# Attention in 80 tile steps placed inside the chunks of two gated convolutions, on one core

## The chip, the core and the metric

One core of a Trainium2 chip runs the whole program. The time is device microseconds from the first to the last instruction. The engines are TensorE (PE, with its weight loads as PEld), VectorE (DVE), ScalarE (ACT), GpSimd (POOL) and SyncE (SP), which only issues transfers. Each runs its own instruction list in order and waits on semaphores.

## What is computed

Windowed attention with a linear bias, then two gated convolution blocks. All data is float32.

```python
# q, k, v: 4 batches, 8 heads, 576 rows, 64 columns; a row sees itself and the 127 rows before it
scores = scale * q @ k.T - slope[h] * distance, masked
attn = exp(scores - max) / (sum + 1e-9);  x = (attn @ v) as (4, 576, 512)
# block 1: 3 taps over h, centred
h = relu(x @ w_in)                        # 512 -> 1024
x = (h * sigmoid(conv3(h))) @ w_out       # 1024 -> 512
# block 2: 5 taps over x, looking back 4 rows
y = ((x @ w_val) * sigmoid(conv5(x))) @ w_out2
```

## The kernel before

The program has two stages, one after the other.

**Attention.** A step is 128 query rows of one pair of heads: 4 batches x 4 pairs x 5 tiles = 80 steps. The fifth tile of a pair (t = 4) has 64 rows only, and the first (t = 0) has fewer keys. A full step is: PE `scores` (L756, two products of 192 columns), DVE `scores` (L582: takes the product out of PSUM, adds the bias and finds the maximum), ACT `exps` (L408, exponential with its sum), DVE `guard` (L596), `invert` (L605) and `normalise` (L614), PE `turn` (L777, four transposes), ACT or DVE `copy_out` (L422, L626), PE `mix` (L808, L805: the product with v). Scores run 5 steps ahead. After a pair's five tiles ACT copies the result from PSUM to `x_all` (L433, L430). The bodies are loops over three batches and one written out.

During this stage POOL takes the twelve 512 KB weight panels, each as it lands: it rounds one into `w_hi` (L345) and subtracts to get `w_lo` (L348), through two buffers `w_raw`.

**The convolutions.** The 2304 rows of x are cut into 8 chunks of 288 rows. For each, PE runs four products, and each block of 128 x 128 weights is used three times (hi x hi, hi x lo, lo x hi, L839 to L841; L893 to L895 in chunk 0): `up` (8 blocks m of 12 products), `val` of the chunk before (4 x 12), `down` (4 x 24), `out` of the chunk before (4 x 12): 288 products. Between `up` and `down` each of the eight blocks m passes ACT `hidden_rows` (L464), DVE three taps (L668, L672), ACT sigmoid (L470), DVE `gated` (L680), ACT rounding to `g1_hi` (L479), POOL subtraction to `g1_lo` (L370). `hidden` and `conv` have DEPTH = 4 buffers, and tap 0 of block m + 1 is issued between taps 1 and 2 of block m. After `down` DVE runs the second block's five taps (L702, L706), and `val_rows` (L690) multiplies by the gate. Before each chunk ACT rounds its 290 columns of `x_all` to `x_hi` (L450) and POOL subtracts (L356). `up` and `down` use PSUM banks 0 to 3, `val` and `out` banks 4 to 7. The first sigmoid needs a load of ACT's function table; the exponential has one at the program's start.

## Time and profile before

| | us |
|---|---|
| median of 3 runs (485.01 to 489.94) | 488.39 |
| span of the profiled execution | 489.8 |
| PE / PEld busy | 453.4 / 415.2 |
| DVE / ACT / POOL busy | 370.8 / 247.8 / 177.9 |

The profile lists instructions with start and duration. A DVE or ACT duration contains some fixed time that overlaps the next instruction, so that the distance between two starts is the better measure of cost. "Idle before" is what the engine stood still, with the name of what ended it. PEclk is the clock that TensorE was granted: 1.00 is its upper level of 2.4 GHz, 0.50 its lower level of 1.2 GHz.

### The profile page before, as it was taken

To read this page: it belongs to the slowest core of one execution; us is meant where nothing else is said; L and a number is where in the kernel's file an instruction comes from. 1 tells how busy PE (TensorE), PEld (TensorE's weight loads), DVE (VectorE), ACT (ScalarE), POOL (GpSimd) and SP (SyncE) were. 2 spreads that over 40 slices of the span, in tenths; PEclk is the share of its full clock that TensorE was granted. 3 is DMA by queue.
4 is the path that set the end of the run, shared out by engine and by line. 5 is a ranking of instruction groups with operands and counts; after the bars stand their busy time and mean duration, and the time that the engine had idled before them with its cause. 6 is when DMAs were issued, how large, how long until landed. Compare 5 with 4: busy or idle time off the path is not lost.

```text
span 489.8 us, 10856 instructions
## 1 busy us (share of the span) xinstructions
PE 453.4 (93%) x3424; PEld 415.2 (85%) x3424; DVE 370.8 (76%) x1078; ACT 247.8 (51%) x746; POOL 177.9 (36%) x181
## 2 busy tenths in 40 slices
PE   4989788887889998999999999999999999999997
PEld 3767566665667897998999999999999999999996
DVE  5889967787767586896696786977968769669750
ACT  3777656775748563354354355255344344435432
POOL 2223522243310026157148136326425605713611
PEclk9999979998879998999999999999999999999999
DMA  5465435433413000000100000010010010010011
GB/s 146 116 176 149 148 106 168 154 115 115 141 49 98 1 2 0 2 1 1 50 1 1 32 17 0 12 36 0 0 48 0 0 48 0 0 48 2 1 48 50
DMA packets 37626, 25.52 MB, mean 52 GB/s; under 512 B 20704, under 2 KB 34016, under 8 KB 37600
## 3 DMA queue, kind: packets, MB, share of 16 engines
q1 hardware_dynamic: 37600, 25.20, 17.1%
q8 instruction: 14, 0.23, 0.2%
q14 instruction: 12, 0.10, 0.1%
HBM read 20.47 MB, written 4.72 MB: 51 GB/s over the span
## 4 chain that ended last, share of the span: by engine, by line
issue 33%; PE 28%; DVE 17%; POOL 16%; ACT 2%; DMA 1%; POOLq 1%; DVEq 0%; SPq 0%; ACTq 0%; PEldq 0%
POOL g_lo L370 10%; PE bank L756 7%; PE bank L777 7%; PE bank L808 5%; DVE guarded L596 4%; POOL x_lo L379 4%; DVE probs L614 3%; DVE conv L672 3%; PE bank L839 2%; PE bank L841 2%; PE bank L840 2%; POOL g_lo L362 2%; DVE gate L706 2%; DVE conv L680 1%; DVE probs L582 1%
## 5 line engine op out<-in xcount | busy, mean ns | idle before, releaser
L839 PE MATMUL bank<-x_hi,w_hi 128*128 128x290 f32 (+1 forms) x384 | 113.8, 296 | 0.5 <-ACT hidden L464 0.5
L840 PE MATMUL bank<-x_lo,w_hi 128*128 128x290 f32 (+1 forms) x384 | 113.7, 296 | 0.0
L841 PE MATMUL bank<-x_hi,w_lo 128*128 128x290 f32 (+1 forms) x384 | 113.7, 296 | 0.0
L839 PE MATMUL bank<-g_hi,w_hi 128*128 128x288 f32 x352 | 105.4, 300 | 3.2 <-POOL g_lo L370 1.7
L370 POOL TENSOR_TENSOR g_lo<-conv,g_hi 128x288 fp32r<-128x288 f32 x64 | 60.2, 949 | 131.2 <-ACT g_hi L479 131.2
L840 PE MATMUL bank<-g_lo,w_hi 128*128 128x288 f32 x352 | 103.9, 295 | 0.0
L841 PE MATMUL bank<-g_hi,w_lo 128*128 128x288 f32 x352 | 103.6, 294 | 0.0
L706 DVE SCALAR_TENSOR_TENSOR gate<-x_all,taps,gate 128x288 f32<-128x288 f32 x128 | 80.7, 630 | 4.5
L672 DVE SCALAR_TENSOR_TENSOR conv<-hidden,taps,conv 128x288 f32<-128x288 f32 x128 | 83.4, 657 | 0.6
L839 PEld LDWEIGHTS bank<-x_hi,w_hi 128*128 128x128 f32 x384 | 72.3, 188 | 0.8 <-ACT hidden L464 0.8
L840 PEld LDWEIGHTS bank<-x_lo,w_hi 128*128 128x128 f32 x384 | 72.8, 189 | 0.0
L841 PEld LDWEIGHTS bank<-x_hi,w_lo 128*128 128x128 f32 x384 | 72.5, 189 | 0.0
L408 ACT ACTIVATE probs<-probs,neg_max 128x192 f32<-128x192 f32 (+1 forms) x144 | 62.1, 434 | 20.2 <-DVE neg_max L582 19.2
L839 PEld LDWEIGHTS bank<-g_hi,w_hi 128*128 128x128 f32 x352 | 66.1, 188 | 6.8 <-POOL g_lo L370 5.7
L582 DVE CUSTOM_DVE_ANT_0 probs<-bank,bias 128x192 f32<-128x192 f32 (+1 forms) x144 | 46.5, 324 | 31.3 <-PE bank L756 22.0
L756 PE MATMUL bank<-k_pair,q_heads 128*128 128x192 f32 (+2 forms) x288 | 63.3, 345 | 6.9 <-DMA k_pair<-k_t 6.9
L777 PE MATMUL bank<-identity,probs 128*128 128x128 f32 x256 | 48.8, 306 | 20.4 <-DVE probs L614 20.2
L841 PEld LDWEIGHTS bank<-g_hi,w_lo 128*128 128x128 f32 x352 | 66.2, 188 | 0.0
L840 PEld LDWEIGHTS bank<-g_lo,w_hi 128*128 128x128 f32 x352 | 66.1, 188 | 0.0
L777 PEld LDWEIGHTS bank<-identity,probs 128*128 128x128 f32 x256 | 28.5, 149 | 35.2 <-DVE probs L614 24.1
L470 ACT ACTIVATE conv<-conv 128x288 f32<-128x288 f32 x64 | 28.5, 445 | 54.8 <-DVE conv L672 54.8
L756 PEld LDWEIGHTS bank<-k_pair,q_heads 128*128 128x128 f32 x288 | 49.4, 214 | 7.0 <-issue 6.8
(55 smaller groups left out, 670.8 us busy)
## 6 DMA issues: line engine op xcount, KB each, us to landing
w_raw<-panels SPq DMA_DIRECT2D x12, 512.0 KB, 4.2
q_heads<-q_t SPq DMA_DIRECT2D x32, 144.0 KB, 3.1
k_pair<-k_t SPq DMA_DIRECT2D x16, 288.0 KB, 3.7
y_t<-y_sb SPq DMA_DIRECT2D x32, 144.0 KB, 1.8
v_pair<-v_pairs SPq DMA_DIRECT2D x16, 256.0 KB, 2.7
v_pair<-v_pairs SPq DMA_DIRECT2D x16, 32.0 KB, 2.5
taps<-taps SPq DMA_DIRECT2D x1, 12.0 KB, 3.6
taps<-taps SPq DMA_DIRECT2D x1, 10.0 KB, 3.9
```

Of the source, the lines that this page charges most:

```text
L370: pool.tensor_tensor(g1_lo[:, m, :], conv[m % DEPTH][:, :], g1_hi[:, m, :], ALU.subtract).then_inc(g1_lo_done, 1)
L408: last = act.activation(probs[r][:, half, lo:hi], probs[r][:, half, lo:hi], ACT.Exp, bias=neg_max[r][:, half:half + 1], scale=-1.0, accum_ ...
L470: act.activation(conv[m % DEPTH][:, :], conv[m % DEPTH][:, :], ACT.Sigmoid).then_inc(gate1_done, 1)
L582: last = dve.tensor_tensor_reduce(probs[r][:, half, lo:hi], s[:, 2 * P * half + lo:2 * P * half + hi], bias_of(hp, t, half), -SCALE, 3e38, ...
L672: dve.scalar_tensor_tensor(out=out, in0=rows, scalar=taps1[:, tap, m:m + 1], in1=out, op0=ALU.mult, op1=ALU.add).then_inc(tap1_done if tap ...
L706: dve.scalar_tensor_tensor(out=out, in0=x2_all[:, m, at + tap:at + tap + HALF], scalar=taps2[:, tap, m:m + 1], in1=out, op0=ALU.mult, op1= ...
L756: last = pe.matmul(s[:, 2 * P * half + lo:2 * P * half + hi], q[:, 2 * t + half, :, :], k[:, first_key + lo:first_key + hi], start=True, s ...
L777: last = pe.transpose(out[:, at:at + P], p[:, half, col:col + P], identity[:, :])
L808: last = pe.matmul(o_ps[hp % 2][rows, t * P:(t + 1) * P], v[:, key_tile, rows], turned_probs, start=(j == 0), stop=(j == blocks - 1))
L839: pe.matmul(out, w_hi[:, p, col:col + P], hi[k], start=first, stop=False)
L840: pe.matmul(out, w_hi[:, p, col:col + P], lo[k], start=False, stop=False)
L841: last = pe.matmul(out, w_lo[:, p, col:col + P], hi[k], start=False, stop=final)
```

## The change

The attention is no longer a stage of its own. Its 80 steps are numbered tile by tile: for each 128 rows of a batch the four head pairs follow one another. The first 12 steps (three tiles) run first. Then every chunk is 24 beats (`up` 8, `val` 4, `down` 8, `out` 4) and before the `down` of chunks 0 to 6 all engines run 8 steps (even chunks) or 12 steps (odd chunks) of attention. Within a run, a slot is PE `turn(s)`, `scores(s + 3)`, then `mix(s - 1)`; DVE `normalise(s + 1)` with guard, reciprocal and product one right after the other, then `scores(s + 3)`; ACT the copy of step s and `exps(s + 2)`. After the fourth pair of a tile ACT rounds the tile from the one PSUM bank `o_ps` into `x_hi`, DVE subtracts into `x_lo`, and the first `mix` of the next tile waits for that. `x_all`, its copies, and POOL's and ACT's separate splits of x are gone.

The convolutions now have PSUM banks 0 to 3 only; the attention has the other four, with one bank instead of two for the transposes. DEPTH is 3. All three taps of a block run one after the other. The weights land in the place of `w_lo` and are split there: six panels by POOL from the start, two among the `g1_low` of chunk 0, and four among its `x2_low`. The query, key and value tiles are loaded per tile of 128 rows for all pairs. `g2` is made in place in `gate2`, and the four rows of history of the second block are copied by POOL. No loop is left: all is written out.

```diff
+LOOK = 3
+RING = LOOK + 1
+V_RING = 3
...
-DEPTH = 4
+BEATS = 24
+VAL0, DOWN0, OUT0 = KW, KW + KM, BEATS - KM
...
+DEPTH = 3
...
+        w_raw_at = top[0]
         w_lo = place("w_lo", [P, PANELS, PANEL], F32R)
-        x_all = place("x_all", [P, BATCH * PAIRS * SEQ])
-        x_hi = place("x_hi", [P, KM, READ], F32R)
-        x_lo = place("x_lo", [P, KM, READ], F32R)
+        w_raw = nc.alloc_sbuf_tensor_at("w_raw", [P, PANELS, PANEL], F32, offset=base + w_raw_at)
...
+        ffn_ps = banks[0:4]
+        s_ps = banks[4:6]
+        t_ps = banks[6]
+        o_ps = banks[7]
...
+        def steps_before(c, j):
+
+
+            if j == DOWN0 and c % 2 == 0 and c < CHUNKS:
+                return range(STEPS * (c // 2) + 12, STEPS * (c // 2 + 1))
+            if j == DOWN0 and c % 2 == 1 and c < CHUNKS - 1:
+                return range(STEPS * (c // 2 + 1), STEPS * (c // 2 + 1) + 12)
+            return range(0)
+
+        def walk(slot, close, beat):
+
+
+            def run(steps):
+                for step in steps:
+                    slot(step)
+                    if step > steps[0]:
+                        close(step - 1)
+                if steps:
+                    close(steps[-1])
+
+            run(range(12))
+            for c in range(CHUNKS + 1):
+                for j in range(BEATS):
+                    run(steps_before(c, j))
+                    beat(c, j)
...
+            def beat(c, j):
+                if c < CHUNKS and 2 <= j < KW + 2:
+                    g1_low(c, j - 2)
+                if c > 0 and 0 <= j - VAL0 - 2 < KM:
+                    g2_low(c - 1, j - VAL0 - 2)
+                if c < CHUNKS and j == VAL0 + 3:
+                    keep_history(c)
+                if c < CHUNKS and j >= DOWN0 + 2 and j < DOWN0 + 2 + 2 * KM and j % 2 == 0:
+                    x2_low(c, (j - DOWN0 - 2) // 2)
+                if c == 0:
+                    for n in {3: (6,), 6: (7,), 14: (8, 9), 18: (10, 11)}.get(j, ()):
+                        split_panel(n)
+
+            for n in range(6):
+                split_panel(n)
+            walk(slot, slot, beat)
...
+            def slot(step):
+                _, t, _ = where(step)
+                cols = 2 * P if t in (0, FULL) else 4 * P
+                act.wait_ge(turned, step + 1)
+
+                reach(act, mixed, step - 1)
+                act.copy(probs_t[step % 2][:, 0:cols], t_ps[:, 0:cols]).then_inc(copied, 1)
+                if step + LOOK - 1 < ALL_STEPS:
+                    exps(step + LOOK - 1)
+
+            def close(step):
+                b, t, hp = where(step)
+                if hp == PAIRS - 1:
+                    w = width_of(t)
+                    act.wait_ge(mixed, step + 1)
+
+                    reach(act, up_done, 2 * KW * b)
+                    act.copy(x_hi[:, :, P * t:P * t + w],
+                             o_ps[:, :].rearrange("p (k s) -> p k s", k=PAIRS)[:, :, 0:w]).then_inc(
+                                 x_hi_done, 1)
...
+            def beat(c, j):
+                if c < CHUNKS and j < KW:
+                    hidden_rows(c, j)
+                if c < CHUNKS and 1 <= j < KW + 1:
+                    gate_rows(c, j - 1)
+                if c > 0 and j < KM:
+                    gate2_rows(c - 1, j)
+                if c < CHUNKS and 2 <= j < KW + 2:
+                    g1_high(c, j - 2)
+                if c > 0 and 0 <= j - VAL0 - 1 < KM:
+                    g2_high(c - 1, j - VAL0 - 1)
+                if c < CHUNKS and DOWN0 <= j < OUT0 and j % 2 == 1:
+                    x2_rows(c, (j - DOWN0) // 2)
+                if c > 0 and j >= OUT0:
+                    out_rows(c - 1, j - OUT0)
...
+                dve.wait_ge(total_guarded, step + 1)
+                dve.reciprocal(inverse[r][:, 0:n], guarded[r][:, 0:n]).then_inc(inverse_done, 1)
+                dve.wait_ge(inverse_done, step + 1)
...
+            def slot(step):
+                if step + 1 < ALL_STEPS:
+                    normalise(step + 1)
+                if step + LOOK < ALL_STEPS:
+                    scores(step + LOOK)
+
+            def close(step):
+                _, t, hp = where(step)
+                if hp == PAIRS - 1:
+                    w = width_of(t)
+                    dve.wait_ge(x_hi_done, step // PAIRS + 1)
+                    dve.tensor_tensor(x_lo[:, :, P * t:P * t + w],
+                                      o_ps[:, :].rearrange("p (k s) -> p k s", k=PAIRS)[:, :, 0:w],
+                                      x_hi[:, :, P * t:P * t + w], ALU.subtract).then_inc(x_lo_done, 1)
+
+            def tap_rows(c, m):
+                n, half = KW * c + m, c % 2
+                rows, out = hidden[n % DEPTH], conv[n % DEPTH][:, :]
+                at = tap_at(half, 0)
+                dve.wait_ge(hidden_done, n + 1)
+
+                reach(dve, g1_lo_done, n - DEPTH + 1)
+                dve.tensor_scalar(out, rows[:, at:at + HALF], taps1[:, 0, m:m + 1], None,
+                                  ALU.mult).then_inc(tap0_done, 1)
+                for tap, before, after in ((1, tap0_done, tap1_done), (2, tap1_done, conv_done)):
+                    at = tap_at(half, tap)
+                    dve.wait_ge(before, n + 1)
+                    dve.scalar_tensor_tensor(out=out, in0=rows[:, at:at + HALF],
+                                             scalar=taps1[:, tap, m:m + 1], in1=out, op0=ALU.mult,
+                                             op1=ALU.add).then_inc(after, 1)
+
...
+            def beat(c, j):
+                if c < CHUNKS and j < KW:
+                    tap_rows(c, j)
+                if c < CHUNKS and 1 <= j < KW + 1:
+                    gated(c, j - 1)
+                if c > 0 and 0 <= j - VAL0 < KM:
+                    val_rows(c - 1, j - VAL0)
+                if c < CHUNKS and DOWN0 + 2 <= j <= OUT0 and j % 2 == 0:
+                    conv2_rows(c, (j - DOWN0 - 2) // 2)
...
+                pe.wait_ge(probs_normal, step + 1)
+                reach(pe, copied, step)
...
+                if hp == 0:
+                    pe.wait_ge(v_loaded[tile % V_RING], 16 * (tile // V_RING + 1))
+
+                    reach(pe, x_lo_done, tile)
+                pe.wait_ge(copied, step + 1)
...
+            def slot(step):
+                turn(step)
+                if step + LOOK < ALL_STEPS:
+                    scores(step + LOOK)
...
+                    pe.wait_ge(x_lo_done, TILES * b + (3 if half == 0 else TILES))
+                    if c == 0:
+                        pe.wait_ge(w_split, P_OUT)
+
+                if m >= KM:
+                    pe.wait_ge(hidden_done, KW * c + m - KM + 1)
+                elif c == 1:
+                    pe.wait_ge(x2_hi_done, m + 1)
+                elif c > 1:
+                    pe.wait_ge(y_kept, KM * (c - 2) + m + 1)
...
+            def beat(c, j):
+                if c < CHUNKS and j < VAL0:
+                    up(c, j)
+                if c > 0 and VAL0 <= j < DOWN0:
+                    val(c - 1, j - VAL0)
+                if c < CHUNKS and DOWN0 <= j < OUT0:
+                    down(c, (j - DOWN0) // 2, (j - DOWN0) % 2)
+                if c > 0 and j >= OUT0:
+                    out(c - 1, j - OUT0)
```

Two places in the lists of instructions. On ACT, the end of chunk 0's eight blocks in the kernel before (g_hi is the rounding of g1, x_hi<-x_all the split of x for the next chunk, x_all<-bank the result of `down`, gate the sigmoid of block 2):

```order
L470 ACTIVATE conv_109<-conv_109 128x288
L479 CAST g_hi<-conv_108 128x288
L479 CAST g_hi<-conv_109 128x288
L450 CAST x_hi<-x_all 128x1160
L510 COPY x_all<-bank 128x288
L511 CAST x_hi<-bank 128x288
```

And the same place in the changed kernel:

```order
L415 ACTIVATE conv_98<-conv_98 128x288
L423 CAST g_hi<-conv_97 128x288
L423 CAST g_hi<-conv_98 128x288
L389 COPY probs_t_84<-bank 128x512
L378 ACT_TABLE_LOAD
L378 ACTIVATE probs_66,total_74<-probs_66,neg_max_70 128x192 x2
L389 COPY probs_t_85<-bank 128x512
```

Behind the last rounding now stands the attention's run: a copy, a table load, and the exponentials of two steps ahead. The next chunk's first sigmoid has a table load too.

On DVE, three blocks of the first convolution before (L668 is tap 0, L672 taps 1 and 2, L680 the gating):

```order
L680 TENSOR_TENSOR conv_106<-hidden_102,conv_106 128x288
L672 SCALAR_TENSOR_TENSOR conv_108<-hidden_104,taps_54,conv_108 128x288
L668 TENSOR_SCALAR conv_109<-hidden_105,taps_54 128x288
L672 SCALAR_TENSOR_TENSOR conv_108<-hidden_104,taps_54,conv_108 128x288
L680 TENSOR_TENSOR conv_107<-hidden_103,conv_107 128x288
```

And now:

```order
L540 TENSOR_SCALAR conv_97<-hidden_94,taps_54 128x288
L545 SCALAR_TENSOR_TENSOR conv_97<-hidden_94,taps_54,conv_97 128x288 x2
L552 TENSOR_TENSOR conv_99<-hidden_96,conv_99 128x288
L540 TENSOR_SCALAR conv_98<-hidden_95,taps_54 128x288
L545 SCALAR_TENSOR_TENSOR conv_98<-hidden_95,taps_54,conv_98 128x288 x2
```

The next block's tap 0 no longer stands between two taps of one block. On POOL, the start of chunk 0's list in the changed kernel, where before only the eight g_lo stood:

```order
L328 TENSOR_TENSOR g_lo<-conv_97,g_hi 128x288
L328 TENSOR_TENSOR g_lo<-conv_98,g_hi 128x288
L320 CAST w_hi<-w_raw 128x1024
L322 TENSOR_TENSOR w_lo<-w_raw,w_hi 128x1024
L328 TENSOR_TENSOR g_lo<-conv_99,g_hi 128x288
```

A panel's split has moved between the blocks of the chunk.

## Rows read from the trace of the kernel before

**Rows 1.** The page's part 1: busy time of each engine.
```profile
PE 453.4 (93%) x3424; PEld 415.2 (85%) x3424; DVE 370.8 (76%) x1078; ACT 247.8 (51%) x746; POOL 177.9 (36%) x181
```
**Rows 2.** Windows: stretch, length, busy of PE, PEld, DVE, ACT, POOL, PEclk, DMA.
```profile
62.00:64.00 2.00, 2.00 (x11) 1.56 (x12) 0.38 (x4) 1.31 (x5) 0.00 (x0) 0.50 0.99 321
140.00:160.00 20.00, 20.00 (x168) 15.31 (x164) 13.34 (x88) 15.12 (x55) 0.00 (x0) 0.93 0.22 61
240.00:280.00 40.00, 39.86 (x298) 39.40 (x296) 30.64 (x57) 18.16 (x48) 16.99 (x17) 1.00 0.05 16
```
**Rows 3.** Chain of waits: start, us, what: the first product of chunks 0, 1; the end.
```profile
166.95 0.33 PE bank L839
...
197.06 0.15 PE bank L895
...
486.82 0.15 PE bank L841
```
**Rows 4.** Timeline, PE: start, us, instruction: the first transposes.
```profile
12.10 0.66 PE L777 MATMUL bank<-identity,probs 128*128 128x128 f32 x2 [0.22 <-DVE probs L614]
```
**Rows 5.** Timeline, POOL and DVE: the split of one weight panel.
```profile
99.45 2.40 POOL L348 TENSOR_TENSOR w_lo<-w_raw,w_hi 128x1024 f32 x1 [0.16 <-POOL w_hi L345]
99.55 2.32 DVE L596 TENSOR_SCALAR guarded<-total 128x2 f32<-128x2 f32 x1
```
**Rows 6.** Timeline, DVE: attention with no panel, and its last steps.
```profile
149.12 0.36 DVE L582 CUSTOM_DVE_ANT_0 probs<-bank,bias 128x192 f32<-128x192 f32 x1 [0.58 <-issue]
...
157.00 0.36 DVE L582 CUSTOM_DVE_ANT_0 probs<-bank,bias 128x192 f32<-128x192 f32 x1 [0.57 <-issue]
...
162.68 0.16 DVE L596 TENSOR_SCALAR guarded<-total 128x2 f32<-128x2 f32 x1
162.87 0.17 DVE L605 RECIPROCAL inverse<-guarded 128x2 f32<-128x2 f32 x1
163.07 0.55 DVE L614 TENSOR_SCALAR probs<-probs,inverse 128x192 f32<-128x192 f32 x2
```
**Rows 7.** Chain of waits: one full step of the attention on PE.
```profile
95.23 0.59 PE bank L777 x4
95.81 0.65 PE bank L756 x4
96.47 0.59 PE bank L808 x8
```
**Rows 8.** Timeline, ACT: the table load of chunk 0.
```profile
172.45 1.28 ACT L470 ACT_TABLE_LOAD   x1
173.75 0.45 ACT L470 ACTIVATE conv<-conv 128x288 f32<-128x288 f32 x1
```
**Rows 9.** Groups by line and form: busy us, mean ns, idle before.
```profile
L408 ACT ACTIVATE probs<-probs,neg_max 128x192 f32<-128x192 f32 x112 | 50.3, 453 | 9.0 <-DVE neg_max L582 7.9
L422 ACT COPY probs_t<-bank 128x512 f32<-128x512 f32 x48 | 28.2, 587 | 26.9 <-PE bank L777 26.6
L690 DVE TENSOR_TENSOR g<-bank,gate 128x288 f32<-128x288 f32 x32 | 14.5, 452 | 21.6 <-POOL g_lo L362 15.2 <-PE bank L841 6.4
```
**Rows 10.** Timeline, DVE: the end of chunk 0's eight blocks, then one chunk.
```profile
185.87 1.42 DVE L680 TENSOR_TENSOR conv<-hidden,conv 128x288 f32<-128x288 f32 x2
...
321.88 0.37 DVE L668 TENSOR_SCALAR conv<-hidden,taps 128x288 f32<-128x288 f32 x1 [3.62 <-ACT hidden L464]
...
328.70 0.45 DVE L680 TENSOR_TENSOR conv<-hidden,conv 128x288 f32<-128x288 f32 x1
...
330.76 0.44 DVE L680 TENSOR_TENSOR conv<-hidden,conv 128x288 f32<-128x288 f32 x1
...
343.44 2.40 DVE L702 TENSOR_SCALAR gate<-x_all,taps 128x288 f32<-128x288 f32 x1 [1.95 <-ACT x_all L510]
...
355.08 2.18 DVE L706 SCALAR_TENSOR_TENSOR gate<-x_all,taps,gate 128x288 f32<-128x288 f32 x4
...
361.11 0.37 DVE L668 TENSOR_SCALAR conv<-hidden,taps 128x288 f32<-128x288 f32 x1 [3.84 <-ACT hidden L464]
```

762 lines of the change are left out of this document (265 added, 497 removed).

## The prediction

> **What bounds the kernel now.** The page's busy times come first. PE is busy for 453 of 489.8 us, DVE for 371, ACT for 248 [rows 1]. A share over the whole span hides that there are two stages, so the windows come next. From 240 to 280 us PE is busy for 39.86 of 40 us with 298 products: the convolutions run at PE's pace of 0.134 us a product, and nobody is waited for [rows 2]. The chain of waits gives the borders. The first `up` starts at 166.95 us, chunk 1 at 197.06, and the last product ends by 487 [rows 3]. Two successive chunks start their taps at 321.88 and 361.11, so that a chunk takes 39.2 us [rows 10]. The span is therefore 167.0 of attention, 30.1 of chunk 0, 7 x 39.2 = 274.6 of chunks 1 to 7, and 18.1 of last `val`, `out` and store.
>
> In the attention the timeline of DVE shows two things. Without a weight panel, five tiles take 157.00 - 149.12 = 7.88 us, 1.58 a step [rows 6], and PE is busy for the whole of that stretch [rows 2]: PE is the bound. A full step is 0.59 + 0.65 + 0.59 = 1.83 us of PE [rows 7]; three of them leave 2.4 us for the two short tiles, 1.2 each. With a panel, DVE's tiny `guard` instruction takes 2.32 us where it takes 0.16 elsewhere, because it stands beside POOL's w_lo subtraction of 2.40 us [rows 5, 6]. The total agrees: from the first turn at 12.1 us [rows 4] to 166.95 are 154.9 us, 80 steps need 126.1, and the 28.8 left are 2.4 for each of twelve panels.
>
> **What the change can take away.** The PE work stays: 80 steps of 1.58 us and 2304 products of 0.134 us are 435 us, in both kernels. The other 55 us of before are the start (12), the panels (29) and the wait of chunk 0 with its lower clock and the tail (some 14). All twelve panels are still split by POOL in the same two instructions. So the change can only hide waits, and the question is what new ones the runs bring. I walk through it from PE's side.
>
> **First run.** 12.1 us to the first turn, as before. Twelve steps are 4 x 1.2 + 8 x 1.83 = 19.4. Five panels fall behind the first turn, at 2.4 each: 12.0. At a tile's border there is a new wait: only one bank holds the result, so the next tile's first `mix` waits for ACT's x_hi and DVE's x_lo. Counted from the new tile's first turn, the old tile's last `mix` ends at 1.83. ACT has a copy (587 ns alone) and two exponentials (453 ns each with their reads) to do [rows 9] and is free at 2.4; x_hi takes it to 3.0. DVE's x_lo reads PSUM as L690 does, at 452 ns for 288 columns [rows 9]; for 512 I take 0.65 (bounds 0.5 and 0.8, with the columns alone or in proportion), so to 3.65. PE wanted to start that `mix` at 1.83 + 0.59 + 0.65 = 3.07: 0.6 lost, and 0.3 more because DVE's next normalise comes late. That makes 0.9 a border (bounds 0.3 and 1.5), twice here. In a tile of short steps DVE and ACT need about 1.45 us a step for the long steps that they work ahead, PE 1.2: 1.0 in all. The last tile's split before `up` can start is open to PE: 1.5. Sum 47.8.
>
> **Chunk 0.** Here DVE is the bound, as before: its eighth gating ended at 185.87 + 1.42 = 187.3, or 20.3 us after `up` began [rows 3, 10]. Blocks followed at 330.76 - 328.70 = 2.06 us [rows 10]. Now no other block's tap stands between two taps of one block, and each of two taps waits for the one before. The distance guard to reciprocal to product of 0.19 and 0.20 us in [rows 6], for instructions of almost no work, shows that such a wait is some 0.1 beyond an overlapped neighbour; I take 0.22 a block, 2.28 us (bounds 2.06 and 2.5). So 1.8 more. Two panels are split among the blocks: 4.8, since a block-2 tap beside a long POOL subtraction took 2.40 us where its like take 0.4 [rows 10]. DVE is done at 26.9. PE has by then had 13.9 us of nothing, as its `up` ends at 12.9 and one turn and one score follow. Then the run's first exponentials need the Exp table again: a load of 1.28 us, with the next activation 1.30 behind the load's start [rows 8]. Last rounding 0.45, copy 0.5, load 1.28, exponentials 1.05, DVE's normalise 0.95: the third turn is at 31.1. Six more steps with one border are 9.4, PE's lower clock after the wait costs 2 (a window such as that in [rows 2], at 0.50, loses half of its length; I take four us of it), `down` is 96 x 0.134 = 12.9. Sum 55.4, against 30.1 + 8 steps of 1.58 before.
>
> **Chunk 1.** Four panels are split among DVE's block-2 taps. These start 3.7 us into `down` (24 products and a copy); four times 0.40 + 2.18 us [rows 10], four panels at 2.4 and four short x2_low at an estimated 0.55 (bounds 0 and their own 0.9) take them to 25.8, which is 12.9 into the next `up`. There DVE is wanted at 2.1. So 10.8 us on top of an odd chunk's normal time.
>
> **Normal chunks.** PE ends `val` at 144 x 0.134 = 19.3 us. DVE starts at 2.1 and is through eight blocks at 19.9 (8 x 2.28, the first two 0.2 shorter as POOL is still idle); four `val_rows` follow. ACT rounds the third of them at 21.5, then copy, load and exponentials to 24.35, and normalise lets the third turn go at 25.4. Without any wait it would go at 19.3 + 2 x 1.83 = 23.0: 2.4 lost at each start of a run. After it come `down` and `out` in 19.3. A chunk with 8 steps is 25.4 + 9.4 + 19.3 = 54.1, one with 12 steps 25.4 + 18.5 + 19.3 = 63.2 (two borders and the short tile in it). Chunks 2, 4, 6: 162.3. Chunks 3, 5: 126.4. Chunk 1: 63.2 + 10.8 = 74.0. Chunk 7 has no run, but its `down` shares banks with `val` and waits for the gating: 39.6. Tail 18.1.
>
> The Sigmoid table's load at the next chunk's start costs nothing here: it stands behind the first `hidden_rows`, while PE makes the second block. If that cover were gone it would be 1.3 us for each of seven chunks. POOL's large x_lo of each chunk goes (it held a tap for 2 us [rows 10]), which is worth nothing, since DVE had 3.6 us idle before the next chunk [rows 10]. The transfers are smaller per request and early; I cost them at nothing, hidden behind 12 steps.
>
> **The sum**: 47.8 + 55.4 + 74.0 + 162.3 + 126.4 + 39.6 + 18.1 = 523.6 us, against 489.8 of the profiled execution. The median of the runs is 1.4 below that, so 522.
>
> Against the change speaks also a rule of the Trainium skill, "ScalarE: Activation LUTs", sections "Table sets: the hidden batching unit" and "What ACT_TABLE_LOAD costs": all calls of one table set should be made before switching, since a switch costs about 2.7 us, a load of 1283 ns and a drain of about as much. The load's length agrees with this case's 1.28 us; the drain does not show in the row, where the load ended 0.02 us before the sigmoid began. By the page the seven Exp loads would cost 1.4 us more each, and the sum would be 533.
>
> **Rivals.** (a) The forecast: waits at starts of runs, at borders and behind panels, 505 to 538 us. Chance 0.78. (b) PE's clock falls at most starts of runs. In [rows 2] a window after such a wait stands at 0.50, the lower level, where all steps take double. Against it: PE comes from 19 us of dense products, and waits here are 1 to 2 us. If six starts each bring a low stretch that costs 3 us, 18 more: 541. Chance 0.12. (c) The other side: DVE is never late. This takes that taps cost no more than 2.06, that the table load falls into a wait, and that POOL's panels do not hold the taps in chunks 0 and 1. It removes the six starts (14.4), chunk 1's lateness (10.8) and 11 in chunk 0: 487, and with borders at 0.3 (7 us less) 480. For it speaks that DVE has the lesser load, 371 busy against 453 [rows 1]; against it, that a tap beside POOL took 2.40 us. It decides from the point where DVE ends its eighth block before PE ends `val`. Chance 0.10, half of it below 484. That the steps simply move without effect on PE (no waits, none hidden) would be 488 and is contained in (c).
>
> **Numbers.** Likeliest 522. The range takes all of (a) and half of (b), 505 to 542. Changes of 1% (4.9 us) are about what a measurement of this kernel can tell from none. Slower by more: (a) and (b), 0.90, less a little for errors that join (a) with (c): 0.88. Within 1%: 0.05. Faster: 0.07.
>
> **What would show it.** In the profile of the changed kernel the first `up` should start near 48 us; chunk 0 should take 50 to 60 us and chunk 1 more than 70; even chunks 54, odd 63. ACT should have seven Exp loads behind the start's, each right before a wait of PE's third turn for DVE's product. PE's idle time should be by the names of `normalise` and, at borders, x_lo. A normal chunk below 52 us, or a period of DVE's blocks of 2.06, would make the forecast too high; PEclk of 0.5 inside the runs, a per-border wait above 1.5 us, or waits on transfers of tiles would make it too low. A cost of fetching a program without loops, which no row here can show, would be on top.

## The result and the profile after

The changed kernel takes 541.45 us (median of 4 runs, 539.47 to 543.65) against 488.97 for the kernel before (485.01 to 489.94). The ratio is 1.1075, 95% interval 1.1005 to 1.1146. It is slower, as forecast, but by 53 us instead of 34: 19 us above the predicted 522 and just inside the upper end of the range. The profiled execution has a span of 541.7 us, against 489.8 before and 523.6 in the sum.

The page's busy times after, and the granted clock in 40 slices of 13.5 us:

```profile
PE 468.2 (86%) x3424; PEld 428.0 (79%) x3424; DVE 392.5 (72%) x1080; ACT 260.9 (48%) x756; POOL 152.9 (28%) x178
...
PEclk9988959979799997999799997999799997799999
```

PE has as many instructions as in [rows 1] and 15 us more busy time: the same work at a lower clock. Of the eight 7s of the PEclk line six are the starts of the runs of attention in chunks 1 to 6. The first is the `up` of chunk 1, which waits for DVE, and the last is a second fall in chunk 6, from the end of its run into `down`. From the first `up` of each chunk to that of the next, the times are these:

| us | forecast | profile |
|---|---|---|
| first run (first `up` at) | 47.8 | 48.65 |
| chunk 0 | 55.4 | 53.75 |
| chunk 1 | 74.0 | 76.7 |
| chunks 2 and 4 | 54.1 each | 57.26 each |
| chunk 6 | 54.1 | 59.17 |
| chunks 3 and 5 | 63.2 each | 65.68, 65.65 |
| chunk 7 and tail | 57.7 | 57.6 |

Chunk 2 shows how a start goes. Its `up` began at 179.12. The timeline of DVE at the end of its eight blocks (start, us, instruction):

```profile
196.44 0.36 DVE L540 TENSOR_SCALAR conv<-hidden,taps 128x288 f32<-128x288 f32 x1
196.83 1.50 DVE L545 SCALAR_TENSOR_TENSOR conv<-hidden,taps,conv 128x288 f32<-128x288 f32 x2
198.25 1.04 DVE L552 TENSOR_TENSOR conv<-hidden,conv 128x288 f32<-128x288 f32 x2
199.21 1.54 DVE L559 TENSOR_TENSOR gate<-bank,gate 128x288 f32<-128x288 f32 x4
200.67 0.16 DVE L507 TENSOR_SCALAR guarded<-total 128x2 f32<-128x2 f32 x1
200.86 0.17 DVE L510 RECIPROCAL inverse<-guarded 128x2 f32<-128x2 f32 x1
201.06 1.36 DVE L514 TENSOR_SCALAR probs<-probs,inverse 128x192 f32<-128x192 f32 x2
```

The timeline of ACT and of POOL in the same stretch:

```profile
200.76 0.58 ACT L389 COPY probs_t<-bank 128x512 f32<-128x512 f32 x1
201.36 1.28 ACT L378 ACT_TABLE_LOAD   x1
202.65 0.46 ACT L378 ACTIVATE probs<-probs,neg_max 128x192 f32<-128x192 f32 x1
...
200.76 1.55 POOL L333 TENSOR_TENSOR g_lo<-gate,g_hi 128x288 fp32r<-128x288 f32 x2
```

And the timeline of PE:

```profile
198.31 0.60 PE L623 MATMUL bank<-identity,probs 128*128 128x128 f32 x4
198.75 0.82 PE L609 MATMUL bank<-k_all,q_tile 128*128 128x192 f32 x4
202.48 0.66 PE L623 MATMUL bank<-identity,probs 128*128 128x128 f32 x4 [2.92 <-DVE probs L514]
202.97 0.49 PE L609 MATMUL bank<-k_all,q_tile 128*128 128x192 f32 x2
203.39 0.66 PE L644 MATMUL bank<-probs_t,v_tile 128*64 128x128 f32 x8
204.68 1.11 PE L623 MATMUL bank<-identity,probs 128*128 128x128 f32 x4 [0.62 <-DVE probs L514]
```

DVE ends its blocks 20.1 us after the start of `up` (forecast 19.9) and the third turn goes at 25.56 (forecast 25.4). The order of events is the one forecast: last rounding, copy, load of 1.28 us, exponentials. But most of what PE stands still is one wait of 2.92 us before the second turn; the third waits only 0.62. The long one ends with DVE's normalise, which takes 1.36 us beside POOL's two g_lo subtractions; without company it takes 0.55, as at 163.07 in [rows 6]. And then the transposes take 1.11 us instead of 0.66. The windows (columns as in [rows 2]) show why:

```profile
200.00:202.00 2.00, 0.00 (x0) 0.00 (x0) 1.93 (x7) 1.98 (x5) 2.00 (x4) 1.00 0.34 77
202.00:204.00 2.00, 1.52 (x14) 1.11 (x14) 1.27 (x7) 1.99 (x6) 1.11 (x3) 1.00 0.71 185
204.00:206.00 2.00, 1.38 (x8) 1.25 (x6) 1.75 (x9) 1.17 (x6) 0.00 (x0) 0.58 0.03 8
206.00:208.00 2.00, 2.00 (x13) 1.31 (x12) 0.95 (x5) 0.86 (x3) 0.00 (x0) 0.50 0.00 0
208.00:210.00 2.00, 2.00 (x13) 1.38 (x11) 0.63 (x4) 1.03 (x3) 0.00 (x0) 0.50 0.00 0
210.00:212.00 2.00, 2.00 (x17) 1.34 (x14) 0.69 (x3) 0.82 (x3) 0.00 (x0) 0.71 0.00 0
```

PE is busy throughout with 13 products in 2 us, and a product takes twice its time: for 6.8 us, from 204.3 to 211.1, PE has its lower level of 1.2 GHz, and somewhat less than half of that, about 3 us, is lost. Chunks 4 and 6 start the same way; in chunks 3 and 5 the wait is 3.26 us and the low stretch, as long, begins before it ends. This is rival (b) of the prediction, in place and in price.

Chunk 1 is late as forecast. DVE's block-2 taps stand beside POOL's splits of four panels (timeline of POOL, then of DVE):

```profile
95.96 2.50 POOL L322 TENSOR_TENSOR w_lo<-w_raw,w_hi 128x1024 fp32r<-128x1024 f32 x1
...
99.75 2.50 POOL L322 TENSOR_TENSOR w_lo<-w_raw,w_hi 128x1024 fp32r<-128x1024 f32 x1
...
99.91 2.51 DVE L568 TENSOR_SCALAR gate<-x_all,taps 128x288 f32<-128x288 f32 x1
102.45 5.70 DVE L572 SCALAR_TENSOR_TENSOR gate<-x_all,taps,gate 128x288 f32<-128x288 f32 x4
...
116.33 0.37 DVE L540 TENSOR_SCALAR conv<-hidden,taps 128x288 f32<-128x288 f32 x1
```

The first tap of chunk 1 starts 13.9 us into its `up` (forecast 12.9; in chunk 2 it is 2.25).

### The profile page after: what moved, and what is told of

Read it like the earlier page. It is cut to its first block, busy times and chain, and to the rows that moved or that the text cites. A ratio compares the mean times of both kernels' runs of the same rounds, so it can differ in the third digit from the quotient of the medians.

```text
span 541.7 us, 9587 instructions
## 1 busy us (share of the span) xinstructions
PE 468.2 (86%) x3424; PEld 428.0 (79%) x3424; DVE 392.5 (72%) x1080; ACT 260.9 (48%) x756; POOL 152.9 (28%) x178
## 4 chain that ended last, share of the span: by engine, by line
PE 51%; DVE 32%; issue 7%; ACT 7%; SPq 1%; DMA 1%; POOLq 0%; POOL 0%; DVEq 0%
DVE conv L545 12%; PE bank L660 10%; PE bank L662 10%; PE bank L661 10%; PE bank L623 7%; PE bank L644 7%; PE bank L609 6%; DVE conv L552 4%; DVE conv L540 4%; DVE gate L572 3%; DVE probs L514 2%; DVE guarded L507 2%; ACT probs L378 1%; ACT L433 1%; DVE gate L559 1%
## 5 line engine op out<-in xcount | busy, mean ns | idle before, releaser
L660 PE MATMUL bank<-g_hi,w_hi 128*128 128x288 f32 x384 | 114.7, 299 | 3.1 <-POOL g_lo L333 1.9
L661 PE MATMUL bank<-g_lo,w_hi 128*128 128x288 f32 x384 | 114.0, 297 | 0.0
L662 PE MATMUL bank<-g_hi,w_lo 128*128 128x288 f32 x384 | 113.9, 297 | 0.0
L623 PE MATMUL bank<-identity,probs 128*128 128x128 f32 x256 | 53.9, 331 | 47.9 <-DVE probs L514 47.8
L572 DVE SCALAR_TENSOR_TENSOR gate<-x_all,taps,gate 128x288 f32<-128x288 f32 x128 | 91.4, 714 | 4.5
L660 PEld LDWEIGHTS bank<-g_hi,w_hi 128*128 128x128 f32 x384 | 72.9, 190 | 4.4 <-POOL g_lo L333 2.1
L609 PE MATMUL bank<-k_all,q_tile 128*128 128x192 f32 (+2 forms) x288 | 69.9, 371 | 5.6 <-DMA k_all<-k_t 5.6
L661 PEld LDWEIGHTS bank<-g_lo,w_hi 128*128 128x128 f32 x384 | 73.0, 190 | 0.0
L389 ACT COPY probs_t<-bank 128x512 f32<-128x512 f32 (+1 forms) x80 | 39.9, 499 | 59.5 <-PE bank L623 59.5
L378 ACT ACTIVATE probs<-probs,neg_max 128x192 f32<-128x192 f32 (+2 forms) x144 | 62.0, 433 | 5.5 <-DVE neg_max L496 5.4
L496 DVE CUSTOM_DVE_ANT_0 probs<-bank,bias 128x192 f32<-128x192 f32 (+2 forms) x144 | 43.0, 331 | 26.4 <-PE bank L609 24.2
```

What stands on the lines that cost most here:

```text
L378: last = act.activation(probs[r][:, half, lo:hi], probs[r][:, half, lo:hi], ACT.Exp, bias=neg_max[r][:, half:half + 1], scale=-1.0, accum_ ...
L389: act.copy(probs_t[step % 2][:, 0:cols], t_ps[:, 0:cols]).then_inc(copied, 1)
L496: last = dve.tensor_tensor_reduce(probs[r][:, half, lo:hi], s_ps[step % 2][:, 2 * P * half + lo:2 * P * half + hi], bias_of(hp, t, half), ...
L572: dve.scalar_tensor_tensor(out=out, in0=x2_all[:, m, tap:tap + HALF], scalar=taps2[:, tap, m:m + 1], in1=out, op0=ALU.mult, op1=ALU.add).t ...
L609: last = pe.matmul(s_ps[step % 2][:, 2 * P * half + lo:2 * P * half + hi], q_tile[tile % 2][:, hp, half, :, :], k_all[:, hp, first_key + l ...
L623: last = pe.transpose(t_ps[:, at:at + P], probs[step % RING][:, half, col:col + P], identity[:, :])
```

## The experiments

Five questions were open: whether the clock is a cause or only an accompaniment; how much the table loads cost; whether the place and the number of the starts matter; what makes chunk 1 late; and what exactly of a panel holds DVE. The kernels ran in three sessions, each beside the kernel before (medians 493.27, 487.84, 491.27 us). So the ratio is what can be compared between them; one hundredth is 4.9 us. Kernels whose names begin with a_ come from the changed kernel, b_ from the one before.

| | us | ratio | 95% interval | first `up` | chunk 1 | chunk 2 | chunk 3 |
|---|---|---|---|---|---|---|---|
| changed kernel | 541.45 | 1.1075 | 1.1005 to 1.1146 | 48.65 | 76.7 | 57.26 | 65.68 |
| a_again | 538.63 | 1.1053 | 1.0965 to 1.1140 | 44.38 | 76.6 | 57.23 | 65.66 |
| a_warm | 524.57 | 1.0663 | 1.0620 to 1.0706 | 45.64 | 75.8 | 54.35 | 63.35 |
| a_half | 534.36 | 1.0859 | 1.0759 to 1.0960 | 45.13 | 76.4 | 54.35 | 64.88 |
| a_tanh | 526.55 | 1.0674 | 1.0644 to 1.0704 | 45.88 | 75.5 | 54.74 | 63.98 |
| a_out | 524.04 | 1.0641 | 1.0599 to 1.0684 | 46.26 | 63.3 | 54.22 | 63.21 |
| a_long | 523.70 | 1.0750 | 1.0691 to 1.0809 | 46.16 | 89.9 | 39.79 | 77.49 |
| a_w8 | 527.53 | 1.0804 | 1.0738 to 1.0869 | 42.01 | 74.8 | 55.31 | 64.53 |
| a_mid | 518.92 | 1.0591 | 1.0477 to 1.0706 | 41.08 | 65.2 | 55.21 | 64.36 |
| a_all | 502.71 | 1.0328 | 1.0272 to 1.0385 | 40.62 | 63.5 | 52.80 | 61.84 |
| b_w8 | 463.15 | 0.9394 | 0.9371 to 0.9418 | 139.09 | | | |
| b_w2 | 482.47 | 0.9800 | 0.9722 to 0.9878 | 158.31 | | | |
| b_w8t | 462.17 | 0.9394 | 0.9326 to 0.9463 | 138.36 | | | |

### The changed kernel again

> The changed kernel once more, unchanged, so that the three variants beside it have their base in the same session. About 1.10 to 1.11 times the kernel before, as measured first. In the earlier session the three variants of this kernel all began their first up at 45.6 to 46.3 us, where the first profile of the changed kernel had 48.65: if that is a difference of sessions, this profile shows 46 too and the total is 2 to 3 us lower against before; if it belongs to the kernel as it is, 48.5 and the ratio 1.107.

The ratio came back at 1.1053. The first `up` is 4.3 us earlier than in the first profile, which neither of the two expectations had. In the first profile PE had 1.2 GHz between 37 and 44 us, which is worth some 3.4 us; here it kept the upper level until 63. The rest isn't more than what varies without it: a_warm and a_half run the same first twelve steps, kept the level too, and began `up` at 45.6 and 45.1. From chunk 1 on the two profiles agree within 0.1 us until chunk 6, which took 59.17 in the one and 56.4 in the other.

### Is it the clock?

a_warm lets PE make 24 idle products while it would wait. They change no result, and DVE ends at the same time as before; only PE isn't still.

```diff
+                if step % STEPS == 12 or (step > 0 and step % STEPS == 0):
+                    pe.wait_ge(scores_kept, step + 3)
+                    for _ in range(WARM):
+                        pe.matmul(s_ps[step % 2][:, 0:P], w_hi[:, 0, 0:P], w_hi[:, 1, 0:P],
+                                  start=True, stop=True)
```

> The changed kernel, with 24 idle products (weights and data from w_hi, 128 columns, into a free scores bank) on PE after the first slot of each of the seven runs inside the chunks, in the 2.9 us in which it waits there. The output is untouched. Theory A (the runs lose about 3 us each because the granted clock falls to 1.2 GHz after that wait, and the steps then take double): the clock stays at 1.00 behind the start of a run, an even chunk goes from 57.3 to about 54 us, an odd one from 65.7 to about 63, and the time from 541 to about 522 us. Rival B (the runs lose their time to DVE and ACT being late, and the low clock only fills waits): within 3 us of 541, with the waits longer by what PE is faster.

The total fell by 4.1 hundredths, 20 us. In the two profiles 17 us of this are in chunks 1 to 6; 3.0 are in the first run, which the idle products don't touch. Against a_again the ratio is 3.9 hundredths lower. The windows of chunk 2's start, which lies 4.96 us earlier than in the profile of the changed kernel, are all at the upper level:

```profile
196.00:198.00 2.00, 1.62 (x16) 1.49 (x15) 1.97 (x6) 1.97 (x3) 2.00 (x4) 1.00 0.61 142
198.00:200.00 2.00, 1.44 (x15) 0.98 (x14) 1.25 (x8) 2.00 (x9) 0.19 (x1) 1.00 0.40 118
200.00:202.00 2.00, 2.00 (x20) 1.53 (x18) 1.60 (x9) 1.15 (x5) 0.00 (x0) 1.00 0.00 0
```

Even chunks take 54.35 and odd ones 63.35 us. The forecast, made without the clock, had 54.1 and 63.2. So the clock was the cause of nearly all of the difference in these chunks, and the rest of their sum stands.

a_half has half as many.

```diff
-WARM = 24
+WARM = 12
```

That leaves a wait of 1.65 to 2.0 us, which is what the prediction had in mind when it called such waits harmless.

> As a_warm, but with 12 idle products of PE instead of 24 after the first slot of each run: they fill about half of the wait of 2.9 us and leave some 1.4 us. The output is untouched. The forecast argued that waits of 1 to 2 us after 19 us of dense products leave the clock up. If that part of the argument holds, and only the length of the wait was misjudged, the granted clock stays at 1.00 in most runs, even chunks take 54 to 55 us as in a_warm, and the total is near a_warm's 1.066 times the kernel before. If a wait of 1.4 us lets the clock fall just as well, even chunks take 56 to 57.3 and the total stays at 1.09 to 1.105.

The result lies between the two theories, because both happened. In chunk 2 the clock stayed up after the wait, in chunk 4 it fell after one that was 0.02 us longer. The second turn of chunk 2, then that of chunk 4 and the window behind it, from the timeline and the windows of a_half:

```profile
198.18 0.66 PE L624 MATMUL bank<-identity,probs 128*128 128x128 f32 x4 [1.65 <-DVE probs L515]
...
317.43 0.66 PE L624 MATMUL bank<-identity,probs 128*128 128x128 f32 x4 [1.67 <-DVE probs L515]
...
320.00:322.00 2.00, 2.00 (x13) 1.56 (x12) 1.31 (x7) 1.03 (x3) 0.00 (x0) 0.50 0.02 4
```

Chunk 2 took 54.35 us, chunk 4 57.23. Of the five starts in chunks 2 to 6, chunks 2 and 5 kept the clock and chunks 3, 4 and 6 had a low stretch behind the start, that of chunk 4 the longest (6.8 us against 3.4). The length of the wait alone doesn't decide it, and what else does was not found. Argued as a certainty, "1 to 2 us are harmless" is wrong as well.

### The function table

a_tanh makes the gates from tanh, which shares a table with the exponential: sigmoid(z) is (1 + tanh(z/2)) / 2, DVE adds the one in the same instruction, and the half goes into the copies after the products. It computes the same gate.

```diff
-                               ACT.Sigmoid).then_inc(gate1_done, 1)
+                               ACT.Tanh, scale=0.5).then_inc(gate1_done, 1)
...
-                dve.tensor_tensor(conv[n % DEPTH][:, :], hidden[n % DEPTH][:, at:at + HALF],
-                                  conv[n % DEPTH][:, :], ALU.mult).then_inc(g1_done, 1)
+                dve.scalar_tensor_tensor(out=conv[n % DEPTH][:, :], in0=conv[n % DEPTH][:, :], scalar=1.0,
+                                         in1=hidden[n % DEPTH][:, at:at + HALF], op0=ALU.add,
+                                         op1=ALU.mult).then_inc(g1_done, 1)
```

> The changed kernel with both sigmoids made from tanh (0.5 + 0.5 tanh(x/2), the halves put into copies and products that are there anyway), which shares ACT's table with the exponential, so that the fourteen table loads inside the chunks are gone. Theory A (a table load is on the path at the start of each run, 1.3 us, as forecast): the third turn of a run comes about 1.3 us earlier, the clock may or may not fall, 541 less 7 to 9 us, about 533. Rival C (each switch costs a drain of another 1.4 us): about 523. Rival B' (the first wait of PE, 2.9 us for DVE, is untouched and hides the load): 541 within 2.

It gave 4 hundredths, 20 us, about twice the seven Exp loads of 1.28 us. The number lies nearer to rival C than to theory A, but the rows bear out neither as it stands. An even chunk is 2.5 us shorter, an odd one 1.7. PE and DVE in chunk 2 of a_tanh, whose `up` starts at 175.25:

```profile
198.20 0.66 PE L628 MATMUL bank<-identity,probs 128*128 128x128 f32 x4 [2.51 <-DVE probs L517]
200.33 1.12 PE L628 MATMUL bank<-identity,probs 128*128 128x128 f32 x4
...
199.04 0.55 DVE L517 TENSOR_SCALAR probs<-probs,inverse 128x192 f32<-128x192 f32 x2
```

The exponentials ahead of this normalise begin 1.86 us earlier after `up` than in the changed kernel: 0.45 for the Sigmoid load, some 1.4 for the Exp load and the gap around it, and no drain of 1.4 us on top. DVE's normalise for the third turn starts 23.8 us after `up` instead of 24.95. So the Exp load was on the path at about its price. The third turn now has no wait, but it comes only 0.48 us earlier (25.08 instead of 25.56), because PE is in a low stretch by then. That stretch, from the second slot's `mix` to the third slot's, is 3.4 us long instead of 6.8, and this is the larger part of the 2.5 us. What shortened it was not found: the wait ahead of it is 2.51 us instead of 2.92, but in a_w8, below, the stretch was as short after 2.91. The 0.4 us off the wait are the Sigmoid load's: in the changed kernel it delays the second block's rows and so DVE's second tap by 0.46 us, which the prediction had put at nothing.

### The place of the runs, and their number

a_out puts each run ahead of `out` instead of ahead of `down`. DVE is then through its blocks long before the run, and `down` waits for the gating instead.

```diff
-            if j == DOWN0 and c % 2 == 0 and c < CHUNKS:
+            if j == OUT0 and c % 2 == 0 and c < CHUNKS:
...
-            if j == DOWN0 and c % 2 == 1 and c < CHUNKS - 1:
+            if j == OUT0 and c % 2 == 1 and c < CHUNKS - 1:
```

> The changed kernel with each run placed before out instead of before down; nothing else is changed. There DVE and ACT have caught up with PE (their work for down is done), so that PE should not wait 2.9 us after the run's first slot. Theory A (place of the run): the start of a run loses only the table load, the clock stays up, down pays 1 to 2 us for the last blocks instead; even chunks 57.3 to 54, odd 65.7 to 63, chunk 1 gains most; sum about 516 to 522. Rival B (any switch between the two kinds of work costs the same wherever it is): 541 within 4.

21 us less. An even run takes 14.38 us on PE instead of 18.96, and `val` with `down` 20.75 instead of 19.34 (a wait of 1.25 us stands there now, and the clock held). Chunk 1 falls to 63.3 but chunk 0 grows to 64.2, so that the two together gain only 3 us.

a_long keeps `down` as the place, but merges the steps of an even chunk with those of the odd one before: 20 steps in chunks 1, 3 and 5, none in 2, 4 and 6.

```diff
-            if j == DOWN0 and c % 2 == 0 and c < CHUNKS:
-                return range(STEPS * (c // 2) + 12, STEPS * (c // 2 + 1))
+            if j == DOWN0 and c == 0:
+                return range(12, STEPS)
...
-                return range(STEPS * (c // 2 + 1), STEPS * (c // 2 + 1) + 12)
+                return range(STEPS * (c // 2 + 1), STEPS * (c // 2 + 2))
```

> The steps of the even chunks are moved to the odd ones: chunk 0 keeps 8, chunks 1, 3 and 5 have 20 each, chunks 2, 4 and 6 have none. The number of starts falls from seven to four; the steps are the same. Theory A (each start of a run costs a wait of 2.4 to 2.9 us and a low stretch of the clock worth 3.2): three starts less are 17 us, from which come one wait of down for the gating in each chunk that has no run now (1.0 each) and one more tile border within a run in each of three (0.9): 541 becomes 528 to 531. Rival (cost goes with the number of steps and not of starts, as it would if each step were longer inside the chunks): no change, 539 to 543.

14.9 us less than a_again, where the theory gave 10 to 13. From the `up` of chunk 1 to that of chunk 7, a_again took 378.8 us and a_long 363.8: 5.0 us net for each of three starts that went, and 5.6 with the 0.6 that a chunk without a run pays for its `down` above 39.2. Not all of it belongs to the starts that went: at the two that stayed in chunks 3 and 5 PE waited 2.8 us instead of 3.26, and behind them it had a low stretch of 3.4 us in chunk 3 and none in chunk 5, instead of 6.8 each. Taken from a_again alone, chunk 2 took 57.23 us against 39.79 without a run and 12.6 for eight steps, 4.8 for its start. So the price of the change goes with the number of starts, not with the number of steps in the chunks.

### Chunk 1 and the panels

a_w8 cuts POOL's subtraction of a panel into eight.

```diff
-                pool.tensor_tensor(w_lo[:, n, :], w_raw[:, n, :], w_hi[:, n, :],
-                                   ALU.subtract).then_inc(w_split, 1)
+                for i in range(8):
+                    part = slice(i * PANEL // 8, (i + 1) * PANEL // 8)
+                    last = pool.tensor_tensor(w_lo[:, n, part], w_raw[:, n, part], w_hi[:, n, part],
+                                              ALU.subtract)
+                last.then_inc(w_split, 1)
```

> POOL's subtraction of each w_lo panel is cut into 8 pieces of 128 columns; nothing else changes. Theory P (DVE is held by the length of one POOL instruction, and the panels make chunk 1 late): guards beside a panel fall below 1 us, the first run loses 8 to 10 of its waits, chunk 0's blocks two long taps of 2.4, and chunk 1 becomes like chunks 3 and 5 (76.7 to about 66), since DVE reaches its first tap within 4 us of up. Together 10 + 4 + 10 less: 541 becomes 515 to 520. Rival Q (DVE is late in chunk 1 for the plain number of its operations and its waits for data, the panels only lying beside them): chunk 1 stays above 72 us and the total above 528.

The gain was 11 us, half of what was expected, and chunk 1 stayed at 74.8, which the expectation had given as the sign of its rival. But the rival's reason isn't it either. The timeline of POOL and of DVE in a_w8:

```profile
94.51 4.85 POOL L324 TENSOR_TENSOR w_lo<-w_raw,w_hi 128x128 fp32r<-128x128 f32 x8
...
108.45 3.33 POOL L324 TENSOR_TENSOR w_lo<-w_raw,w_hi 128x128 fp32r<-128x128 f32 x8
111.74 0.79 POOL L341 TENSOR_TENSOR x_lo<-x_all,x_hi 128x288 fp32r<-128x288 f32 x1
112.49 1.56 POOL L331 TENSOR_TENSOR g_lo<-conv,g_hi 128x288 fp32r<-128x288 f32 x2
...
99.60 0.91 DVE L543 TENSOR_SCALAR conv<-hidden,taps 128x288 f32<-128x288 f32 x1
...
113.40 0.82 DVE L543 TENSOR_SCALAR conv<-hidden,taps 128x288 f32<-128x288 f32 x1 [5.93 <-POOL g_lo L331]
```

DVE reached chunk 1's first tap 4.65 us into `up` instead of 13.9. Where DVE and POOL work side by side, eight pieces take POOL 4.85 us, against 2.50 for the whole. With the rounding ahead of it a panel is up to 6 us, and four of them stand in POOL's queue before the last x2_lo and the first g1_lo of chunk 1. Now POOL is late: `val` begins at 112.58, and the fourth block waits 5.93 us for a buffer that g1_lo frees. The lateness had only changed engines. The first run gained 2.4 us, not the 8 to 10 expected: its waits were not the panels alone.

a_mid is a_w8 with those four panels where POOL has nothing to do.

```diff
-                    for n in {3: (6,), 6: (7,), 14: (8, 9), 18: (10, 11)}.get(j, ()):
+                    for n in {3: (6,), 6: (7,), 11: (8, 9, 10, 11)}.get(j, ()):
```

> The kernel a_w8 (w_lo in 8 pieces) with one more edit: POOL splits panels 8 to 11 between its last g1_lo of chunk 0 and the run, where it had 18 us of nothing, instead of among chunk 0's four x2_lo. In a_w8 chunk 1 still took 74.85 us, and its waits were for POOL: four panels of 6 us each stood ahead of the last x2_lo (111.74 us) and of the first g1_lo (112.49). Theory (chunk 1 is late because of where the four panels stand, whichever engine they make late): chunk 1 falls to 64 to 66 us like chunks 3 and 5 (64.5 in a_w8), chunk 0 grows by at most 3 for panels beside the run, and the total falls by 7 to 10 from 527.5 to about 519. Rival (chunk 1 is late by something of the first pass, such as its taps or its values): chunk 1 stays above 72 and the total at 526 to 529.

Chunk 1 took 65.2 us, close to chunk 3's 64.4, and chunk 0 grew by 1.3. Beside the run, a panel's pieces take 3.37 to 3.58 us. So chunk 1's 10 us do come from where the four panels stand.

### What of a panel holds DVE

b_w8 is the kernel before with the same eight pieces.

> The kernel before the change, with POOL's subtraction of a weight panel made in eight pieces of 128 columns instead of one of 1024. Theory A (the twelve panels cost the attention 2.4 us each because a DVE instruction beside the whole subtraction waits for its end): with pieces of 0.3 us DVE gets between them and the first stage ends 15 to 25 us earlier, 489 to about 468. Rival B (the loss is by POOL's total time at work, not by the length of one instruction): the guard's mean stays near 0.5 us and the time within 4 us of 489.

6.1% faster than the kernel before, and 15% faster than the changed one. The first `up` starts at 139.09 us instead of 166.95 [rows 3], which is 12.1 and 80 steps of 1.58 (138.2 together) within a microsecond: all that the twelve holds cost is gone, though POOL now needs 3.4 to 3.6 us for a panel instead of 2.40. The clock is 0.996 in the mean. The timeline of POOL and of DVE beside one panel, to be laid beside [rows 5]:

```profile
63.63 3.40 POOL L350 TENSOR_TENSOR w_lo<-w_raw,w_hi 128x128 f32 x8 [0.16 <-POOL w_hi L345]
...
63.82 0.81 DVE L618 TENSOR_SCALAR probs<-probs,inverse 128x192 f32<-128x192 f32 x2
64.55 0.14 DVE L600 TENSOR_SCALAR guarded<-total 128x1 f32<-128x1 f32 x1
...
65.82 0.41 DVE L600 TENSOR_SCALAR guarded<-total 128x2 f32<-128x2 f32 x1
```

The windows from the first turn to the first `up`, in the kernel before and in b_w8 (columns as in [rows 2]), show what the holds had cost:

```profile
12.10:166.90 154.80, 134.60 (x1105) 101.91 (x1105) 121.34 (x591) 105.16 (x374) 43.49 (x25) 0.93 0.41 122
12.10:139.10 127.00, 124.32 (x1105) 94.50 (x1105) 108.92 (x591) 103.64 (x374) 56.53 (x109) 1.00 0.50 148
```

PE stood still for 20.2 us before and for 2.7 now, so a panel made PE wait 1.5 us, not 2.4. The other 10.3 of the 27.8 us are the same 1105 instructions at a lower clock: the kernel before already paid for the clock behind such waits.

b_w2 has two pieces of 512 columns.

> The kernel before with POOL's w_lo subtraction in 2 pieces of 512 columns (b_w8 had 8 of 128 and won 29 us, which is all of the twelve holds of 2.4). Theory L (DVE is held until the one POOL instruction that runs has ended): each hold is at most 1.2 to 1.3 us, twice a panel if a DVE instruction of the held kind meets both pieces. DVE has about 0.2 us of slack in a step of 1.58, so that most of it is still lost if both pieces are met: between 462 + 12 x 1.0 = 474 (one met) and 486 (both). Rival C (it is the number of columns that POOL works on, not the length of one instruction, so that any cut gives the same): 463.

The first `up` is at 158.31 us: with the low clock in it, 1.6 us are lost for each panel, where the whole lost 2.3 and eight pieces 0.1. DVE meets both pieces. A normalise is two instructions, one of them ran into each piece (timeline of POOL and of DVE):

```profile
66.64 2.50 POOL L350 TENSOR_TENSOR w_lo<-w_raw,w_hi 128x512 f32 x2 [0.16 <-POOL w_hi L345]
...
66.88 2.34 DVE L618 TENSOR_SCALAR probs<-probs,inverse 128x64 f32<-128x64 f32 x2
```

b_w8t adds the tanh gates to b_w8.

> The fastest so far, b_w8 (the kernel before with w_lo in 8 pieces), with the gates from tanh instead of sigmoid, so that the program needs one function table. Same gates. Before had one load of 1.28 us, in chunk 0, where PE waits for DVE and ACT. Theory: at most 1.3 us less than b_w8's 463, 461 to 463 and not separable from it, since only one load goes. In the changed kernel the same edit gave 15 us because it had fourteen. Rival (tanh, or the products with one added, are themselves faster or relieve DVE): 5 us or more less.

462.17 us, in another session and at the same ratio to the kernel before as b_w8. The one table load that goes is not worth a measurable amount where the program switches once.

### All together

a_all has the tanh gates, the runs ahead of `out`, and the eight pieces.

> Three edits at once on the changed kernel: the gates come from tanh (one function table for the whole program), the runs stand before out instead of before down, and w_lo is subtracted in 8 pieces. Measured alone, the first gave 15 us and the second 17, against 541; both take the same wait at the start of a run and the low clock behind it, so that together they should give 20 to 24. With 20 to 25 for the pieces the total is 492 to 500, about the kernel before, but well behind the kernel before with its w_lo in pieces (463 in the earlier session). If the costs left are none but these, it ends near 490; if it stays above 505, something else than starts and panels costs inside the chunks.

502.71 us: 36 us less than a_again and 3.3% slower than the kernel before. Even chunks take 52.80 us, which is 39.2 and eight steps of 1.58 (51.8 together) and one more. Odd ones take 61.84 where the same count gives 58.2. What is left above the count is in chunk 0 (57.1 against 30.1 and 12.6 for its steps, 42.7), chunk 1, and the borders of tiles in the runs. The page's PEclk shows dips in the first 100 us and then almost none. It didn't reach the 492 to 500 that was expected, and it is 9.3 hundredths, 46 us, behind b_w8.

## Why the prediction came out as it did

**What bounds before, and where gains could be**: the size was right, the reading in part. The 28.8 us put down to twelve holds of 2.4 are 17.5 us of waits and 10.3 of low clock, as b_w8 shows; together they were worth 26 to 29 us. b_w8 won these by cutting one instruction; the change moved the panels to places where they hold other work.

**First run, 47.8**: 48.65 in the profile, 44.38 in the control. So the agreement within a microsecond is luck: some 3.4 us of the profile's are a low stretch that the term hadn't. Two terms were off and hid each other. The first turn came at 13.88 instead of 12.1, since DVE's first `guard` now stands behind its wait for the taps, of 3.6 us. And five panels at 2.4 on the path were too much: cutting them gave 2.4 us in all.

**The border's x_lo, 0.65 to 0.69**: 0.69 us as recorded. The new tile's first `mix` waited 0.54 to 0.64 us (forecast 0.6; 1.09 in chunk 6), and `up` after the first run 1.41 (forecast 1.5). The whole price of a border, 0.9, was not measured by itself; that the chunks with the clock held came out at 54.35 and 63.35 bounds its error.

**Chunk 0, 55.4**: 53.75. The panels' two long taps were there (2.50 and 2.44 us), and DVE was through at 25.7 instead of 26.9. The clock was at 0.50 from 67.8 to 81.4 us, 5.4 us of it with PE at work again. The forecast had allowed for four, and here alone.

**Period of DVE's blocks, 2.28**: 2.18 to 2.35 in chunk 2, end of the eighth at 20.1 against 19.9.

**Table loads**: on the path for Exp, 1.28 us, as costed; the Sigmoid load, put at nothing, cost DVE 0.46 us. Weighed against the sum was the Trainium skill, "ScalarE: Activation LUTs", section "What ACT_TABLE_LOAD costs", whose switch of about 2.7 us would have added 1.4 to each. The row of the load ends at 202.64 and the exponential begins at 202.65, and the third turn came 0.16 us after the forecast that had no such drain. The trace doesn't bear out the drain; the same page's advice to batch by table set, in "Table sets: the hidden batching unit", is borne out by a_tanh, with 20 us for it, more than half of it by way of the clock.

**Chunk 1, 10.8 us of lateness**: right in mechanism and place, 13.9 against 12.9 into `up`. a_mid shows it.

**Chunk 7 and tail, 57.7**: 57.6, by luck. The 18.1 had been what was left over in the trace before, where chunk 1 in truth took 41.3 us, not 39.2, and the tail 16.6. In the changed kernel the tail grew by 1.2 us, and the chunk without a run took 39.8 instead of 39.6.

**The failed step: the dismissal of rival (b).** "PE comes from 19 us of dense products, and waits here are 1 to 2 us." Both halves failed. The wait is 2.9 us in even and 3.3 in odd chunks. The sum's 2.4 was counted from a third turn at 23.0, with two whole steps of PE ahead of it; but a run's first slot has no `mix`, the rows give 22.0, and PE stands still 3.5 us though the third turn comes as forecast. Most of that falls ahead of the second turn, where POOL's short g2_lo subtractions hold the normalise for 0.8 us, which no term had. And 19 us of dense work ahead didn't keep the clock: in the row at 204 it is down. a_half shows that even 1.67 us can be enough. The missing term is the 3 us that the rival had as its price: 3.2 in chunks 2 and 4, 5.1 in chunk 6, where the clock fell a second time ahead of `down`, 2.5 in 3 and 5, 2.7 in chunk 1: 19 us in all, and the sum misses the profile by 18.1.

With the clock held a_warm gives back 17.0 of the 19; what is left is 1.8 us of chunk 1's 2.7 and at most 0.3 in any other. So 541.45 lies in the range of 505 to 542 only because half of rival (b) had been taken into it. The forecast's own case (a), with a chance of 0.78, ended at 538 and did not hold; (b), at 0.12, is what happened, and its 541 was right.

The trace of before held the warning. [rows 2] has a window at 0.50, and the forecast didn't look at how long the wait ahead of it was. It was 1.69 us. Of the seven waits of 1.5 to 1.9 us in that stage four had a low stretch at their end or within 2 us of it; another of 1.87 left the clock at 1.00 (timeline of PE, kernel before):

```profile
61.03 1.12 PE L777 MATMUL bank<-identity,probs 128*128 128x128 f32 x4 [1.69 <-DVE probs L614]
...
93.33 0.44 PE L777 MATMUL bank<-identity,probs 128*128 128x128 f32 x2 [1.87 <-DVE probs L614]
```

Rival (c), DVE never late, had 0.10 and failed in every chunk; its condition, DVE through before `val` ends, is what a_out makes true by the place of the run.

## What to carry to other kernels

Before moving work to hide a wait between two engines, look at what one instruction of the other engine holds, and cut it: eight pieces cost POOL a microsecond a panel and gave the whole program 6%. Where a change makes PE stop for 1.5 us or more at several places, put a low stretch of the clock behind each into the sum as a case of its own (here about 3 us behind most waits of 2.9), and prefer few starts to many. And after taking one engine's lateness away, read the other queue: the eight pieces that freed DVE made POOL late by the same amount.
